# Attention with one score pass: probabilities turned on TensorE, first loads and transfers on two queues

## The reference

```python
q_bits = (np.einsum('bhsd,dk->bhsk', q, proj) > 0).astype(np.int64)
...
mask = q_bucket[:, :, :, None] == k_bucket[:, :, None, :]
scores = scale * np.matmul(q, k.transpose(0, 1, 3, 2))
scores = np.where(mask, scores, -1000000000.0)
scores = scores - np.max(scores, axis=-1, keepdims=True)
attn = np.exp(scores)
attn = attn / (np.sum(attn, axis=-1, keepdims=True) + 1e-09)
return np.matmul(attn, v).astype(np.float32)
```

## Time and profile before

| what | value |
|---|---|
| median of 3 runs | 598.43 us (595.02 to 602.29) |
| the profiled execution: its time, its span | 599.8 us, 598.0 us |
| PE busy | 514.6 us, 86% |
| DVE, ACT, POOL busy | 324.3, 307.9, 146.6 us |
| PE, ten slices of 14.95 us from the start | 2282999999 |
| PEclk, the same ten slices | 9997999999 |
| DMA | 79.44 MB, 56352 packets |

### The profile page before, as it was taken

How to read it: one execution, slowest core, us unless ns; L and a number is a source line. 1 busy time by engine, 2 the same in 40 slices (tenths; PEclk the granted TensorE clock), 3 DMA queues, 4 the chain that set the end, 5 groups by cost and what they waited for, 6 DMA issues and landing times.

```text
span 598.0 us, 7261 instructions
## 1 busy us (share of the span) xinstructions
PE 514.6 (86%) x2666; PEld 324.1 (54%) x2666; DVE 324.3 (54%) x452; ACT 307.9 (51%) x468; POOL 146.6 (25%) x98
## 2 busy tenths in 40 slices
PE   2282999999999999999998685678869798998996
PEld 1261656565565656565555221222358586886875
DVE  0173466555556565555533520112789988888860
ACT  1072566667666766676653310000636666766750
POOL 6247030303012030300000000004223454554541
PEclk9997999999999999999998897886979999999998
DMA  8887534547873597246003939996000001001001
GB/s 177 175 271 177 112 85 103 126 97 251 197 162 85 120 336 153 56 101 206 1 2 126 420 142 394 399 382 246 0 1 0 0 2 71 1 0 70 0 0 71
DMA packets 56352, 79.44 MB, mean 133 GB/s; under 512 B 29112, under 2 KB 33592, under 8 KB 55680
## 3 DMA queue, kind: packets, MB, share of 16 engines
q1 hardware_dynamic: 56320, 79.01, 44.8%
HBM read 54.59 MB, written 3.15 MB: 97 GB/s over the span
## 4 chain that ended last, share of the span: by engine, by line
PE 64%; DVE 13%; SPq 7%; DMA 7%; issue 4%; ACT 3%; POOL 1%; DVEq 0%; POOLq 0%
PE unit L293 38%; PE o_acc L293 21%; DMA w<-in_moe_w 6%; SPq L337 3%; DVE nmax L636 2%; PE unit L849 2%; DVE fu L793 2%; DVE g L804 1%; DVE halves L684 1%; SPq L346 1%; PE unit L979 1%; SPq L314 1%; PE unit L938 1%; DVE fe L788 1%; ACT probs L521 1%
## 5 line engine op out<-in xcount | busy, mean ns | idle before, releaser
L293 PE MATMUL unit<-op 128*128 128x512 f32 (+1 forms) x768 | 167.8, 357 | 26.0 <-DMA op<-bit 23.8
L293 PEld LDWEIGHTS unit<-op 128*128 128x128 f32 x768 | 120.9, 193 | 73.8 <-issue 50.6
L636 DVE TENSOR_REDUCE nmax<-unit 128x1 f32<-128x768 f32 x96 | 91.6, 956 | 121.9 <-PE unit L293 121.9
L513 ACT ACTIVATE unit<-unit,nmax 128x768 f32<-128x768 f32 x96 | 84.0, 875 | 102.9 <-DVE nmax L636 102.5
L488 POOL TENSOR_TENSOR g_lo<-g,g_hi 128x1024 fp32r<-128x1024 f32 x24 | 73.0, 3042 | 91.3 <-ACT g_hi L593 91.3
L521 ACT ACTIVATE probs<-unit 128x768 f32<-128x768 f32 x96 | 77.9, 811 | 16.3 <-PE unit L293 15.5
L293 PE MATMUL o_acc<-probs,vn 128*64 128x384 f32 x384 | 83.8, 515 | 1.2 <-DMA vn<-in_v 1.1
L445 POOL TENSOR_SCALAR hi<-qk_t 128x768 fp32r<-128x768 f32 x16 | 13.3, 831 | 175.3 <-ACT qk_t L506 175.3
L293 PE MATMUL unit<-wo_hi,g_hi 128*128 128x512 f32 x96 | 39.1, 407 | 12.4 <-DVE m_pack L782 5.5
L478 POOL TENSOR_SCALAR wo_hi<-wo_raw 128x2048 fp32r<-128x2048 f32 x4 | 9.1, 2295 | 158.9 <-PE unit L293 158.5
L804 DVE TENSOR_TENSOR g<-fv,fr 128x1024 f32<-128x1024 f32 x24 | 45.4, 1890 | 4.2 <-ACT fr L602 4.1
(11 more groups left out here) (139 smaller groups left out, 641.9 us busy)
## 6 DMA issues: line engine op xcount, KB each, us to landing
w<-in_moe_w SPq DMA_DIRECT2D x16, 2048.0 KB, 11.6
op<-hi SPq DMA_DIRECT2D x48, 192.0 KB
w_in_sb<-in_moe_w_in SPq DMA_DIRECT2D x1, 4096.0 KB, 18.2
wo_raw<-in_moe_w_out SPq DMA_DIRECT2D x2, 2048.0 KB, 17.6
qn<-in_q SPq DMA_DIRECT2D x16, 192.0 KB, 3.9
kn<-in_k SPq DMA_DIRECT2D x16, 192.0 KB, 3.9
op<-lo SPq DMA_DIRECT2D x16, 192.0 KB
op<-lo SPq DMA_DIRECT2D x32, 96.0 KB
```

The lines of the kernel that those rows point to most:

```text
L293: return nc.tensor.matmul(out_, lhsT, rhs, start=start, stop=stop, skip_group_check=True)
L513: sc.activation(s, s, ACT.Exp, bias=nmax[:, g % 4, t:t + 1], accum_out=sums[:, g % 4, t:t + 1]).then_inc(sum_done, 1)
L636: ve.tensor_reduce(nmax[:, g % 4, t:t + 1], unit("M", i)[:, 0:S], AX.X, ALU.max, negate=True).then_inc(max_done, 1)
```

## The change

Scores are computed once. Per tile: product S (with queries in the rows), row maximum on DVE, two small DVE instructions on it (`keep` is 0 or 1 and `shift` the negative maximum, or both 0 for a row without a partner), and one exponential on ACT that writes `probs` and the row sums. Then PE turns the tile with six transposes (P), and ACT (two tiles of three) or DVE (the third) copies it to `turned`, from which `weigh` reads 384 columns at a time. The second product E, the rows R, the value totals V and `lv` go. S runs two tiles ahead of P. `op` has three places in place of four. A head is spread by 8 DMAs and not by 12 or 13. For the first head the key loads, one set of constant rows and half of the spreading are issued by ACT's queue, and the first low parts are cut on DVE.

```diff
-    LEAD = 9
+    LEAD = 2
...
+    UNITS = [("T", 0), ("T", 1), ("H", 0), ("T", 2), ("T", 3), ("S", 0), ("S", 1)]
...
+        todo = [("P", T * h + s)]
         prep = (h + 3) // 2 if h % 2 == 1 else NP
         if prep < NP and s < 2:
             todo.append(("T", 2 * prep + s))
         if prep < NP and s == 3:
             todo.append(("H", prep))
...
-        todo.append(("E", T * h + s))
-        if s == 3 and h > 0:
+        if s == 4 and h > 0:
             todo.append(("F", h - 1))
         if T * h + s + LEAD < T * G:
-            todo.append(("M", T * h + s + LEAD))
+            todo.append(("S", T * h + s + LEAD))
...
+        PLACES = 3
+        def spread_query_high(eng, g):
+            n, b, head = g // 2, op[g % PLACES], slice(D * (g % 2), D * (g % 2) + D)
+            eng.wait_ge(hi_done, 2 * n + 1)
+            eng.dma_start(b[0:D, QA:QB + 1, :].bitcast(F32),
+                          cuts[head, 0:1, :].bitcast(F32).broadcast_to([D, 2, S])).then_inc(ops_in[g % PLACES], 16)
...
             def spread(g):
...
-                if g >= 4:
-                    sp.wait_ge(pv_done, 6 * (g - 3))
+                if g >= PLACES:
+                    sp.wait_ge(keys_done, T * (g - PLACES + 1))
+                spread_query_high(sp, g)
+                for half in range(2):
+                    spread_crossed(sp, g, half)
+                spread_key_parts(sp, g)
+                for x in range(2):
+                    spread_bits(sp, g, x)
...
+            spread(2)
+            spread(3)
+            load_qk(2)
+            load_v(1)
...
-            for n in range(1, NP):
+            for n in range(2, NP):
+                spread(2 * n)
+                spread(2 * n + 1)
                 if n + 1 < NP:
                     load_qk(n + 1)
-                spread(2 * n)
-                spread(2 * n + 1)
-                if n >= 2:
-                    load_v(n)
+                load_v(n)
...
+            def exponentials(i):
+                g, t = i // T, i % T
+                act.wait_ge(shifted, i + 1)
+                if i >= 3:
+                    act.wait_ge(p_turned, i - 2)
+                sc.activation(probs[i % 3][:, :], unit("S", i)[:, 0:S], ACT.Exp, bias=shift[:, g % 4, t:t + 1],
+                              scale=keep[:, g % 4, t:t + 1], accum_out=sums[:, g % 4, t:t + 1]).then_inc(exp_done, 1)
+            def copy_probs(i):
+                act.wait_ge(p_turned, i + 1)
...
+            for h in range(2):
+                act.dma_start(kn[0][:, :, h, :], k_h[:, h, :, :]).then_inc(qk_in[0], 16)
+            act.wait_ge(const_rows, 1)
+            load_const_rows(act, 0)
+            copy_turned(0)
+            copy_turned(1)
+            spread_key_parts(act, 0)
+            spread_crossed(act, 0, 1)
+            copy_turned(2)
+            copy_turned(3)
+            spread_bits(act, 0, 1)
...
+            def row_max(i):
+                ve.tensor_reduce(nm, unit("S", i)[:, 0:S], AX.X, ALU.max, negate=True).then_inc(max_done, 1)
+                dve.wait_ge(max_done, i + 1)
+                ve.tensor_scalar(keep[:, g % 4, t:t + 1], nm, -MASKED, 0.0, ALU.is_lt, ALU.add)
+                ve.scalar_tensor_tensor(out=shift[:, g % 4, t:t + 1], in0=nm, scalar=-MASKED, in1=nm,
+                                        op0=ALU.is_lt, op1=ALU.mult).then_inc(shifted, 1)
...
+            def turn_probs(i):
+                u = claim("P", i)
+                pe.wait_ge(exp_done, i + 1)
                 for t in range(T):
+                    f = slice(t * P, (t + 1) * P)
+                    ins = nc.tensor.transpose(u[:, f], probs[i % 3][:, f], ident[:, :])
+                ins.then_inc(p_turned, 1)
```

More of the change, by code:

```diff
@@ L122, in build_program @@
         QA, QB, KA, KB = range(4)
-        op = [sb(f"op{n}", [P, 4, S], F32R, at=e_at if n < 2 else None) for n in range(4)]
-        hi = sb("hi", [P, 2, S], F32R, at=e_at)
-        lo = sb("lo", [P, 2, S], F32R)
+        PLACES = 3
+        op = [sb(f"op{n}", [P, 4, S], F32R, at=e_at if n < 2 else None) for n in range(PLACES)]
+        cuts = sb("cuts", [P, 4, S], F32R)
         bit = sb("bit", [P, HS], F32R)
         vn = [sb(f"vn{n}", [P, 2, T, D]) for n in range(2)]
-        probs = [sb(f"probs{n}", [P, S]) for n in range(4)]
+        probs = [sb(f"probs{n}", [P, S], at=e_at if n < 2 else None) for n in range(3)]
+        turned = [sb(f"turned{n}", [P, T, 3, P]) for n in range(2)]
         ot = sb("ot", [P, S])
-        zero_rows = sb("zero_rows", [P, S])
-        lv = sb("lv", [P, G * D], F32R)
         hash_w = sb("hash_w", [P, 32])
-        ones_f = sb("ones_f", [P, 1])
         nmax = sb("nmax", [P, 4, T])
+        keep = sb("keep", [P, 4, T])
+        shift = sb("shift", [P, 4, T])
         sums = sb("sums", [P, 4, T])
[L136 to L139, removed]
         den = sb("den", [P, T])
@@ L349, in _ @@
-            load_qk(0)
+                if g >= PLACES:
+                    sp.wait_ge(keys_done, T * (g - PLACES + 1))
+                spread_query_high(sp, g)
+                for half in range(2):
+                    spread_crossed(sp, g, half)
[3 more added lines that the diff above has]
+            for h in range(2):
+                sp.dma_start(qn[0][:, :, h, :], q_h[:, h, :, :]).then_inc(qk_in[0], 16)
             sp.wait_ge(hash_clear, 1)
@@ L353, in _ @@
             load_qk(1)
+            spread_query_high(sp, 0)
+            spread_crossed(sp, 0, 0)
+            spread_bits(sp, 0, 0)
             sp.wait_ge(const_rows, 1)
-            for b in range(4):
-                load_const_rows(b)
-            spread(0)
+            load_const_rows(sp, 1)
             spread(1)
-            sp.dma_start(v_all[:, :, :, :], v_h[:, :, :, :]).then_inc(v_all_in, 16)
             load_v(0)
+            load_const_rows(sp, 2)
+            spread(2)
+            spread(3)
+            load_qk(2)
             load_v(1)
@@ L382, in _ @@
                 if n == 5:
-                    sp.wait_ge(v_totalled, 1)
                     load_w1(1)
@@ L913, in weigh @@
-            def weigh(pair, half):
-                h, j = pair // 3, pair % 3
-                bank = o_acc[:, 512 * half:512 * half + HS]
-                cols = slice(HS * half, HS * (half + 1))
-                pe.wait_ge(exp_done, 2 * pair + 2)
-                if j == 0 and h >= 1:
-                    pe.wait_ge(o_copied, 2 * (h - 1) + half + 1)
-                if j == 0 and h % 2 == 0:
-                    pe.wait_ge(v_in[h // 2 % 2], 32 * (h // 4 + 1))
+                product(u, op[g % PLACES], QA, KA, t).then_inc(keys_done, 1)
@@ L962, in _ @@
             for h, s in SLOTS:
-                for kind, i in slot_units(h, s):
-                    in_order(kind, i)
-                if 3 * h + s // 2 >= 1:
-                    weigh(3 * h + s // 2 - 1, s % 2)
-            for half in range(2):
-                weigh(3 * G - 1, half)
+                i = T * h + s
+                for kind, n in slot_units(h, s):
+                    in_order(kind, n)
+                if i >= 3:
+                    weigh(i // 3 - 1, i % 3)
+            for j in range(3):
+                weigh(2 * G - 1, j)
             turn_out(G - 1)
```

332 lines of the change are left out of this document (128 added, 204 removed).

## The result

The changed kernel takes 621.48 us, the median of 4 runs (619.76 to 622.02), and the kernel before 598.02 us beside it (4 runs, 595.02 to 602.29). The ratio is 1.0399, with a 95% interval of 1.0361 to 1.0438: slower by 4.0%. The forecast was 601 with a range of 582 to 614, so the time lies outside the range, 7.5 us above its upper end.

A forecast was written before the change was run, and what follows sets the result against it. PE was taken to bound the attention. A gain of 23.8 us up to the first transposes of pair 2 and a loss of 25.4 after gave net +1.6 on 599.8: forecast 601 us, range 582 to 614.

The forecast's parts named there:

- A spread is then 4 x 0.71 + 4 x 0.70 + 0.1 = 5.7: SP's queue: issuing one head's eight spread DMAs takes 5.7 us, two-column DMAs priced like the old one-column ones.
- the bound of 7.7: SP's queue: upper bound in us for issuing a spread, with the large DMAs at 1.21 each.
- The rival at 614: SP's queue: two-column DMAs issue at 1.21 each, chain 13.8 us long, total 614 us; chance 13%.
- T4: First transposes of pair 2 on PE, in slot 0 of head 1: forecast at 45.0 us, before at 68.82.
- load waits, pairs 3 to 7: PE stands still for late query and key loads at these pairs' transposes: 5 x 4.7 = 23.5 us.
- clock, six waits: PE's clock falls to half in each wait for late loads, costing 2.3 us each: 13.8 us.
- wait at H (with the part ahead of P): PE's wait at the buffer claim in slots with extra unit H: 0.2 us each, six times.
- P with an extra unit behind it: PE's six transposes turning a tile, priced at 0.64 us per slot at full clock.
- the chain of 2.4: End of a score product, through maximum, keep, shift and exponential, to release of PE's next weight load: 2.4 us.
- In 32 in heads 13 to 15.: Attention's last heads: sign that the forecast is right, two heads taking 32 us there.
- loads in time: Rival: query and key loads arrive without making PE wait, total 560 us; chance 8%.
- the case of 808 us: Rival: PE's clock stays at half through the attention, each 2.30 us slot doubles, total 808 us; chance 2%.

The follow-up runs named there:

- the loads ahead: Changed kernel with only load_qk(n+1) put back ahead of spread(2n), and load_qk(2) ahead of spread(2): 572.34 us, ratio 0.9597 to the kernel before.
- the filled wait: Changed kernel with 24 identity products on PE ahead of each waiting transpose of next queries and keys: 611.68 us, ratio 1.0267 to the kernel before.

## Why the prediction was wrong

The mechanism was right: one edit in SP's queue decides, six waits stand at the T of pairs 2 to 7, each with a fall of the clock. The experiment with the loads ahead shows it from one side (ratios 1.0399 and 0.9597 to the kernel before, 8% apart), the same edit in the kernel before from the other. The wrong step is "A spread is then 4 x 0.71 + 4 x 0.70 + 0.1 = 5.7". It measured 7.85, just above the bound of 7.7 that I had set from the earlier trace rows. The rival at 614, given 13%, came nearest, but partly by luck: it had the four large DMAs at 1.21 each, and they took 0.70 to 0.92 (3.4 in all, 0.5 above the forecast), while the bits took 4.24 instead of 2.80. I priced the bits at 0.70, from a place in the earlier trace rows where the data ahead of them was nearly through. I kept the duration of the issue apart from the data that it puts on the way. Behind the large parts, 1.2 MB issued in 3.5 us, the small DMAs are issued more slowly; with a quarter of that data a spread takes 5.9, and pairs 6 and 7 wait the 4.7 that I had forecast.

By the terms of the sum, up to the attention end (323.5 forecast, 348.99 measured, 25.5 apart):

| term | forecast | measured | difference, us |
|---|---|---|---|
| T4 | 45.0 | 51.68 | +6.7 |
| load waits, pairs 3 to 7 | 5 x 4.7 = 23.5 | 33.8 | +10.3 |
| clock, six waits | 6 x 2.3 = 13.8 | 6 x 1.7 | -3.6 |
| wait at H (with the part ahead of P) | 6 x 0.2 | 6 x 1.3 or so | +6.6 |
| P with an extra unit behind it | 0.64 | 0.72 to 0.80 | +3 |
| not resolved | | | +2.5 |

- **Load waits.** Chain of 14.0 instead of 11.8; the 2.2 are the 2.15 of the issue, and the fourth load was priced rightly.
- **T4.** The same step again, twice: `spread(1)` was issued in 9.8 us (17.04 to 26.85) and `spread(3)` in 8.0 (37.68 to 45.66), each forecast at 5.7, together 6.4 of the 6.7. The first is in the chain because POOL's cut of pair 1 (28.20) waits for the bits of `spread(1)`, and `spread(2)` for POOL; it ended at 37.59, not at 33. The product S5, which `spread(3)` also waits for, was 2.9 late as well (done at 36.2, forecast 33.3), so a faster `spread(1)` alone need not have won its whole 4.1. The first product came 1.6 later than forecast.
- **Clock.** It fell in the waits as forecast, but less work than I had put stands at the low level: 1.2 or 2.3 in turn by the rows up to the S behind the second T, 1.7 in the mean and by the filled wait, not 2.3.
- **H.** The wait of 1.36 is not in the chain of 2.4 that I had added up from the earlier trace rows, since DVE's instruction for `shift` was priced from a one-operand row. The trace of before held the sign, in a row that I did not look for: a 128x6 instruction on two tiles, 2.21 us long at 46.91, while POOL worked.
- **Right as forecast.** The slot of 2.30 (the S at 112.77 and the next at 115.07), the wait of 0.4 behind F (109.45 to 110.44 is 0.99, forecast 0.6 + 0.4), ACT and DVE not the bound outside the slot of H, and the transposes at full clock.
- **"In 32 in heads 13 to 15."** Heads 13 to 15, without T and H, ran at 14.93 each, 29.9 for two. The prediction's own terms give 29.6 (12 slots, two F with their waits), so the 32 was a slip and the slot was priced rightly. But with T, H and F two heads take 35.0 without any load wait, where the terms give 30.8 + 1.8 = 32.6. That is no less than before, so the product that was taken away bought no time in the dense part. The forecast of 560 for the case "loads in time" was 12 too low: six times 2.4 is already more, T4 came 2.8 later than the 39.3 of that case, and what won the rest back is not resolved.

Of the second stage, 4.8 us shorter in this execution, I can name 1.6 (the transposes at 348.99 took 5.46, those of the earlier trace rows 7.04, in part at half clock). It varied from 269.6 to 276.3 between executions, and the rest stays open.

## What to carry to other kernels

A load's place in a queue is to be judged by what the DMA ahead of it waits for: here moving four DMAs behind one semaphore wait cost 8% of the kernel, twice the 4.0% that the rest of the change gained. When a queue's issues are priced from rows, take rows with the same amount of data on the way, and keep the pessimistic bound in the sum if there are none. When a small instruction sometimes takes ten times its usual length, look at what the other engines do beside it; here it was POOL.

## What the runs showed of the hardware

- **Issuing slows down behind data.** DMAs of 9 KB are issued in 0.70 us each when they go first and in 1.06 right behind the large parts of a spread (1.2 MB issued in 3.5 us, DMA engines full at 200 to 215 GB/s); with a quarter of that data 0.74; and a load of keys took 2.10 instead of 0.65 when it was the one behind. Full engines alone do not do it: the kernel before issued high parts in 0.62 each at a DMA share of 0.98. What in the queue sets the pace is not shown.
- **DVE waits for POOL on two-operand instructions.** A 128x1 instruction with two tiles in SBUF takes 1.31 us (up to 1.78) while POOL runs TENSOR_TENSOR, ends when POOL does, and takes 0.15 in the median; the same computation with one tile operand takes 0.20 to 0.21 always, beside POOL too. The Trainium skill (GPSIMD Engine Reference, section 1: Specifications) gives GpSimd's SBUF interface as shared with VectorE, with contention for DVE instructions with two SBUF inputs: the traces agree.
- **Transposes run at full clock.** In the kernel with the loads ahead six transposes stand in each slot of 2.30 us, beside products, and the granted clock is 1.00 (2.4 GHz) in every 40 us of 40 to 280. The stronger sign is the earlier trace rows, where it rises from 0.50 to 1.00 while transposes alone run. The Trainium skill (TensorE: Matmul & The Clock Gate, Part 4: PE-mode transpose) has them not engage it; these traces disagree, and the case of 808 us did not come.
- **A second issuing queue at the start** gave a first product at 20.91, one queue 19.16.
